# Value products of the rest tiles by chunk with both column halves side by side, and one-row products last in a transform piece

## The chip, the cores and the metric

The kernel runs on one core of one Trainium2 chip. The metric is the device time of one execution in microseconds, lower is better. The kernel before takes 1379.33 us, the median of three runs (1378.09 to 1381.95).

## What is computed

The reference chains three layers on float32 data, for a batch of 4, 8 heads, 576 tokens, a head dimension of 64 and a model dimension of 512:

```python
scores = q @ k.T / 8                      # top 32 scores of each row are kept, the rest masked
attn   = exp(scores - max) masked, divided by its row sum
x      = attn @ v                         # (4, 576, 512) after the heads are joined
mixed  = real(fft over width (fft over tokens (x)))
u      = x + mixed
un     = layer_norm(u);  x2 = u + relu(un @ w_ch1) @ w_ch2
xn     = layer_norm(x2) * g_ln;  out = x2 + relu(xn @ w2_ch1) @ w2_ch2
```

## The kernel before, in words

The order of all work is written out by hand in **slots** `s`. Each of the 144 slots below `TILES` handles one score tile; 36 of them (`NT`) make one batch element `b`. Per slot TensorE transposes the masked exponentials of its tile (`probs_T`, L667), computes later scores (L625, L619), and, where a tile closes a pair, multiplies probabilities by values (`values`). After slot 39 the two-layer MLP is woven in: a unit is one 128-wide slice of the hidden layer, with `mlp1` (L719) and `mlp2` (L736). From slot 144 on only MLP units and the last batch element's transform are left.

VectorE finds the 32nd largest score of each row (`pair`: four rounds of MAX8, L1109, and three of MATCH_REPLACE8, L1115, for two tiles at a time, then the masking multiply L1122), and the next pair starts when the last is done. ScalarE copies PSUM out, computes the exponentials (L902), and issues the loads of scores that were set aside (`sc_ahead`). `probs_T(s)` waits for the mask of its tile; `exps` of a later pair stands behind `probs_out(s)` in ScalarE's order. So VectorE waits for TensorE through ScalarE, and TensorE waits for VectorE at L667.

576 tokens are four full chunks of 128 and a **rest** of 64. Most tiles hold 128 query rows. A **rest tile** (`tile_of(i)` gives chunk `CF`) holds the 64 rest rows of two heads, one head in each half of the partitions. There is one for each pair of heads and batch element, 16 in all, in slots 8, 9, 26, 27 of each batch element's 36: slots 8, 9, 26, 27, 44, 45, 62, 63, 80, 81, 98, 99, 116, 117, 134 and 135. Its value products (L684) take the probabilities as weights, 64 columns for one head, and the values as the moving operand, 65 columns (64 and a column of ones, which yields the row sum). The output `PV` has head 0 in partitions 0 to 63 and head 1 in 64 to 127: each product fills one **column half** of the array. The loop is over heads outside and the five chunks inside, and the fifth chunk is cut to its 64 rows, `pT[0:w]` and `vn[0:w]`. Below those rows `ex` holds zeros (a memset of columns 576 to 639), so `pT` does too, and `vn` holds ones there.

All other tiles use L690, which goes by chunk outside and head inside; its weights are `vn` with 64 columns, its moving operand `pT` with 128 columns, and its output also has one head in each column half.

The transform over tokens and width comes in `PIECES` = 10 pieces per batch element (`dft_piece`): 0 to 3 over tokens (L763, L770), 4 to 9 over width (L775, L779), two for each of three blocks of rows `j`. For batch elements 1 and 2 a piece has two sides of 129 columns, for 0 and 3 one side of 258. Even width pieces (4, 6, 8) add the alternating term, a product with a single contraction row (L779), between the two full products of each side. Pieces come two to a slot: for b = 1 the pieces 4, 6, 8 are in slots 80, 81, 82, for b = 2 in 118, 119, 120, for b = 3 in 152, 153, 154. The even piece stands ahead of `values(s)`, the odd one behind `mlp2`. For b = 0 all pieces come in one burst in slot 37. The third block has 64 rows, so its weights have 64 columns.

In the trace each of these float32 products is two records of a weight load and two of a matmul (transposes are one each), so L684 has 10 products and 20 matmul records for each rest tile.

Of the kernel before, what the change touches and what calls it, by code (L numbers as in the profile page):

```python
# [8 lines left out]
P = 128  # L9
CF = S // P  # L10
TAIL = S - CF * P
C = CF + 1
# [123 lines left out]
def width(c):  # L136

    return P if c < CF else TAIL


def tile_of(i):

    block, r = divmod(i, 2 * TPP)
    if r < 2 * CF:
        return 2 * block, r // 2, r % 2
    if r < 2 * CF + 2:
        return 2 * block + r - 2 * CF, CF, None
    return 2 * block + 1, (r - 2 * CF - 2) // 2, r % 2


def first_tile(hp):

    return hp // 2 * 2 * TPP + (TPP if hp % 2 else 0)


def chunk(b, c):

    return b // 2 * 2 * CF + b // 2 + (2 * CF if c == CF else b % 2 * CF + c)


def piece_slot(b, i):

    if b == 0:
        return SEAM
    return {1: 78, 2: 116, 3: 148}[b] + i // 2
# [42 lines left out]
def build(nc, q, k, v, g2, w_raw, seq_t, wid_t, alt_t, w_low, sc_ahead, out):  # L208
# [4 lines left out]
    with ctx:  # L213
        def sb(name, shape, dt=f32):
            return ctx.enter_context(nc.sbuf_tensor(name, shape, dt))
# [13 lines left out]
        alt = sb("alt", [1, EO])  # L229
        gb = sb("gb", [P, DM])  # L230
        vn = sb("vn", [P, 2, C, 2, D + 1])
# [8 lines left out]
        pT = sb("pT", [P, 2, C * P])  # L240
# [7 lines left out]
        aT = sb("aT", [P, 4, SO])  # L248
# [23 lines left out]
        PV = Tp[:, C * P:C * P + D + 1]  # L272
# [94 lines left out]
        def rest(b):  # L367

            return slice(TAIL * (b % 2), TAIL * (b % 2 + 1))
# [5 lines left out]
        def piece_cols(b, i):  # L375

            total = SO if i < 4 else EO
            return 2 if 0 < b < B - 1 else 1, total // 2 if 0 < b < B - 1 else total

        def piece(b, i):  # L380

            rows = piece_rows(b, i)
            sides, n = piece_cols(b, i)
            if b == 0:
                bank = Ac[rows, i % 4, :] if i % 4 < 3 else Hp[rows, :]
                return bank[:, 0:n].unsqueeze(1)
            if b < B - 1:
                return Sp[rows, :, HALF:HALF + n]
            return Sp[rows, 1, 0:n].unsqueeze(1)
# [215 lines left out]
        def _(pe):  # L605
# [64 lines left out]
            def values(s):  # L670
                b, i = divmod(s, NT)
                hp, t, head = tile_of(i)
                par = hp % 2
                if head == 0:
                    return
                if i <= first_tile(hp) + 1:
                    pe.wait_ge(s_v[par], 3 * 16 * ((NHP // 2) * b + hp // 2 + 1))
                pe.wait_ge(s_pT_sb, s + 1)
                if t == CF:
                    for h in range(2):  # L680
                        o = slice(h * TAIL, (h + 1) * TAIL)
                        for c in range(C):
                            w = width(c)
                            last = nc.tensor.matmul(PV[o, :], pT[0:w, i % 2, c * P + o.start:c * P + o.stop],  # L684
                                                    vn[0:w, par, c, h, :], start=(c == 0), stop=(c == C - 1))
                    last.then_inc(s_pv_ps, 1)
                    return
                for c in range(C):
                    for h in range(2):
                        last = nc.tensor.matmul(OT[h * D:(h + 1) * D, :], vn[:, par, c, h, 0:D], pT[:, h, c * P:(c + 1) * P],  # L690
                                                start=(c == 0), stop=(c == C - 1))
                last.then_inc(s_pv_ps, 2)
# [50 lines left out]
            def dft_piece(b, i):  # L743
                if i == 0:
                    pe.wait_ge(s_fold, b + 1)
                    if b in (1, 2):
                        pe.wait_ge(s_rem, b)
                if b == 0:
                    if i == 0:
                        pe.wait_ge(s_ah_sb, AHEAD)  # L750
                    if i >= 4:
                        pe.wait_ge(s_pc_sb, max(4, i - 3))
                else:
                    pe.wait_ge(s_pc_sb, PIECES * b + i)
                    if b < B - 1:
                        pe.wait_ge(s_sc_sb, min(piece_slot(b, i) + RING + 1, KEPT))
                where, (sides, n) = piece(b, i), piece_cols(b, i)
                for side in range(sides):
                    o, col = where[:, side, :], slice(side * n, (side + 1) * n)
                    if i < 4:  # L760
                        for kc in range(J):
                            r = slice(0, P) if kc < HP else rest(b)
                            last = nc.tensor.matmul(o, xf[r, kc, i // 2, (i % 2) * P:(i % 2 + 1) * P], seq[r, i // 2, kc, col],  # L763
                                                    start=(kc == 0), stop=(kc == J - 1))
                            if i == 2 and kc == 0:

                                for km in range(J):
                                    r = slice(0, P) if km < HP else rest(b)
                                    mid = xs[:, 0, km, FOLD:FOLD + 1] if km < HP else U[r, chunk(b, CF), FOLD:FOLD + 1]
                                    nc.tensor.matmul(o[0:1, :], mid, seq[r, 0, km, col], start=False, stop=False)  # L770
                    else:
                        j, part = divmod(i - 4, 2)
                        to = slice(j * P, j * P + (P if j < HP else TAIL))
                        for kk in range(2):
                            last = nc.tensor.matmul(o, aT[:, 2 * part + kk, to], wid[:, part, kk, col],  # L775
                                                    start=(kk == 0), stop=(kk == 1))
                            if part == 0 and kk == 0:

                                nc.tensor.matmul(o, aT[0:1, 2, to], alt[0:1, col], start=False, stop=False)  # L779
                last.then_inc(s_pc_ps, 1)  # L780

            def un_T(t):
# [26 lines left out]
            for s in range(SLOTS):  # L809
# [19 lines left out]
                if s != SEAM and pieces:  # L829
                    dft_piece(*pieces[0])  # L830
                if s < TILES:
                    values(s)
                for n in closing_at(s):
                    mlp2(n)
                if s != SEAM and pieces:
                    dft_piece(*pieces[1])
# [7 lines left out]
                if s == SEAM:  # L844
                    pe.wait_ge(s_tab, 48)
                    for b, i in pieces:
                        dft_piece(b, i)
# [511 lines left out]
```

## Time and profile before

| | |
|---|---|
| median of three runs | 1379.33 us (1378.09 to 1381.95) |
| profiled execution, its own time | 1380.66 us |
| its span | 1378.9 us |
| TensorE matmul busy | 1271.3 us (92%), 7944 records |
| VectorE busy | 1113.0 us (81%) |
| ScalarE busy | 789.3 us (57%) |
| GpSimd busy | 348.8 us (25%) |
| chain that ended last | TensorE 62%, VectorE 30% |
| mean granted clock of TensorE | 0.971 of full |

How to read it: busy shares are averages over stages that differ, so a saving on TensorE counts only in a stage in which TensorE is what the others wait for. In the rows, `128*64 128x65` means 128 contraction rows by 64 weight columns, and a moving operand of 65 columns. A row of the timeline joins records of one line that follow each other; its time runs from the first start to the last end.

### The profile page before, as it was taken

Reading aid. Unit: us, or ns where it says so; the run is one execution under the profiler, and the core shown is the slowest. Engines: PE = TensorE matmul, PEld = TensorE weight load, DVE = VectorE, ACT = ScalarE, POOL = GpSimd, SP = SyncE. Lnnn points to the kernel's source line nnn. Section 1 sums busy time; section 2 is a strip of 40 time slices with the busy share of each in tenths; the row PEclk is TensorE's granted clock in tenths of the full one; section 3 lists DMA queues with packets and bytes.
Section 4 is the critical chain, followed back from the end, with each engine's and each line's share of the span. In section 5 each row is a group of like instructions: output and inputs, shape, how many; then the busy total and the mean of one; then the engine's idle time right before and its main releaser. Section 6 shows DMA issues by size and latency. Waiting matters only on the chain.

```text
span 1378.9 us, 22760 instructions
## 1 busy us (share of the span) xinstructions
PE 1271.3 (92%) x7944; PEld 1037.2 (75%) x7944; DVE 1113.0 (81%) x2224; ACT 789.3 (57%) x1564; POOL 348.8 (25%) x308
## 2 busy tenths in 40 slices
PE   5877778999999699799998999999999999999999
PEld 2444444777777578688887788888689999999998
DVE  7999999999999988999889789975485555555553
ACT  4777765677777456575665556654344434444442
POOL 3444430122122341132233222322121121212110
PEclk8998989999999999999999999999999999999999
DMA  7899993566757656787786467663244343333342
GB/s 258 310 339 340 328 340 129 186 218 207 245 180 257 191 187 216 247 272 237 231 281 225 155 230 243 218 229 131 76 165 143 121 156 120 130 123 123 122 146 84
DMA packets 117396, 280.63 MB, mean 204 GB/s; under 512 B 29730, under 2 KB 29731, under 8 KB 117283
## 3 DMA queue, kind: packets, MB, share of 16 engines
q1 hardware_dynamic: 105522, 231.98, 51.0%
q10 hardware_dynamic: 10368, 42.47, 8.1%
q0 software_dynamic: 1392, 4.73, 1.0%
q8 instruction: 65, 1.06, 0.3%
q14 instruction: 49, 0.39, 0.1%
HBM read 235.87 MB, written 42.73 MB: 202 GB/s over the span
## 4 chain that ended last, share of the span: by engine, by line
PE 62%; DVE 30%; issue 4%; POOL 1%; ACT 1%; DMA 1%; SPq 0%; DVEq 0%; ACTq 0%; POOLq 0%
PE Big L736 24%; PE Big L719 17%; DVE top L1109 13%; DVE wk L1115 12%; PE Sp L719 7%; PE Tp L667 3%; DVE ex L1122 3%; PE Tp L690 2%; PE Sp L763 2%; PE Tp L684 1%; PE Sp L775 1%; DVE st L1201 1%; PE Tp L794 1%; PE Sp L625 1%; PE Big L763 1%
## 5 line engine op out<-in xcount | busy, mean ns | idle before, releaser
L736 PE MATMUL Big<-wr,hh 128*128 128x512 f32 x1152 | 362.6, 396 | 0.0
L719 PE MATMUL Big<-uh,wr 128*128 128x256 f32 (+1 forms) x1384 | 317.2, 319 | 7.4 <-ACT hh L963 7.4
L1109 DVE MAX8 top<-wk 128x8 f32<-128x576 f32 x432 | 304.4, 746 | 0.0
L719 PEld LDWEIGHTS Big<-uh,wr 128*128 128x128 f32 x1384 | 233.0, 191 | 26.8 <-issue 18.7
L736 PEld LDWEIGHTS Big<-wr,hh 128*128 128x128 f32 x1152 | 217.9, 189 | 41.7
L736 PE MATMUL Big<-wr,hl 128*128 128x512 f32 x576 | 238.3, 414 | 3.6 <-DVE wr L1254 2.6
L500 POOL TENSOR_TENSOR hl<-hf,hh 128x256 fp32r<-128x256 f32 (+1 forms) x123 | 105.3, 856 | 471.7 <-ACT hh L963 471.6
L719 PE MATMUL Big<-ul,wr 128*128 128x256 f32 (+1 forms) x692 | 215.5, 311 | 0.0
L1115 DVE MATCH_REPLACE8 wk<-top,wk 128x576 f32<-128x576 f32 x288 | 211.5, 741 | 0.0
L667 PE MATMUL Tp<-ident,ex 128*128 128x128 f32 x720 | 120.8, 295 | 50.5 <-DVE ex L1122 46.7
L909 ACT ACTIVATE pT<-Tp 128x640 f32<-128x640 f32 x144 | 101.4, 704 | 112.3 <-PE Tp L667 112.0
L667 PEld LDWEIGHTS Tp<-ident,ex 128*128 128x128 f32 x720 | 89.7, 150 | 94.1 <-issue 60.7
L963 ACT ACTIVATE hh<-Big 128x256 fp32r<-128x256 f32 (+1 forms) x173 | 74.6, 431 | 119.1 <-PE Big L719 119.1
L1122 DVE SCALAR_TENSOR_TENSOR ex<-sc,top,ex 128x576 f32<-128x576 f32 x144 | 119.7, 869 | 25.6 <-ACT ex L902 25.6
L719 PEld LDWEIGHTS Big<-ul,wr 128*128 128x128 f32 x692 | 132.5, 192 | 0.0
L736 PEld LDWEIGHTS Big<-wr,hl 128*128 128x128 f32 x576 | 108.8, 189 | 31.1 <-issue 10.8
L1109 DVE MAX8 top<-sc 128x8 f32<-128x576 f32 x144 | 101.6, 747 | 20.5 <-DMA sc<-sc_ahead 13.5
L1115 DVE MATCH_REPLACE8 wk<-top,sc 128x576 f32<-128x576 f32 x144 | 105.7, 741 | 0.0
L902 ACT ACTIVATE ex<-sc,nmx 128x576 f32<-128x576 f32 x144 | 103.9, 769 | 2.3
L494 POOL TENSOR_TENSOR wr<-wf,wr 128x1024 fp32r<-128x1024 f32 x32 | 75.3, 2369 | 111.3 <-DVE top L1109 110.6
L719 PE MATMUL Sp<-uh,wr 128*128 128x384 f32 (+1 forms) x408 | 99.9, 329 | 0.0
L962 ACT ACTIVATE hf<-Big 128x256 f32<-128x256 f32 (+1 forms) x123 | 50.8, 413 | 74.2 <-PE Big L719 74.2
(133 smaller groups left out, 1859.3 us busy)
## 6 DMA issues: line engine op xcount, KB each, us to landing
wf<-in_weights SPq DMA_DIRECT2D x206, 512.0 KB, 3.6
wr<-w_low SPq DMA_DIRECT2D x246, 256.0 KB, 4.3
sc<-in_weights SPq DMA_DIRECT2D x50, 512.0 KB, 3.3
sc<-sc_ahead ACTq DMA_DIRECT2D x36, 576.0 KB, 5.5
w_low<-wr SPq DMA_DIRECT2D x32, 512.0 KB, 6.5
sc_ahead<-U ACTq DMA_DIRECT2D x18, 576.0 KB, 4.7
sc_ahead<-un ACTq DMA_DIRECT2D x9, 576.0 KB, 4.0
sc_ahead<-yb ACTq DMA_DIRECT2D x9, 576.0 KB, 6.3
```

What stands on the lines that cost most here:

```text
L494: pool.tensor_tensor(wr[:, r, :, 1, :], wf[:, j % WFS, :, :], wr[:, r, :, 0, :].bitcast(f32), ALU.subtract).then_inc(s_wlow, 1)
L500: pool.tensor_tensor(hl[:, n % 2, 0:w], hf[:, n % 2, 0:w], hh[:, n % 2, 0:w].bitcast(f32), ALU.subtract).then_inc(s_hl[0], 1)
L667: last = nc.tensor.transpose(Tp[:, c * P:(c + 1) * P], ex[:, s % RING, c * P:(c + 1) * P], ident[:, :])
L719: last = nc.tensor.matmul(hidden(n), a[:, kd * P:(kd + 1) * P], x[:, kd, 0:P * SIZE[p]], start=(kd == 0 and j == 0), stop=(kd == KD - 1 an ...
L736: last = nc.tensor.matmul(Ac[:, j, :], a[:, n % 2, j * P:(j + 1) * P], w, start=(f == 0 and m == 0), stop=(f == KF - 1 and m == 2))
L902: nc.scalar.activation(ex[:, s % RING, 0:S], sc[:, s % RING, :], ACT.Exp, bias=nmx[:, s % RING:s % RING + 1], scale=1.0 / np.sqrt(D)).then ...
L909: nc.scalar.activation(pT[:, s % 2, :], Tp[:, 0:C * P], ACT.Copy).then_inc(s_pT_sb, 1)
L962: nc.scalar.activation(hf[:, n % 2, 0:w], hidden(n), ACT.Relu)
L963: nc.scalar.activation(hh[:, n % 2, 0:w], hidden(n), ACT.Relu).then_inc(s_h_sb, 1)
L1109: nc.vector.max(top[:, s % RING, r, :], src).then_inc(s_top, 1)
L1115: nc.vector.match_replace(out=wk[:, a, :], in_to_replace=top[:, s % RING, r, :], in_values=src, imm_value=STRUCK).then_inc(s_struck, 1)
L1122: nc.vector.scalar_tensor_tensor(out=ex[:, s % RING, 0:S], in0=sc[:, s % RING, :], scalar=top[:, s % RING, ROUNDS - 1, 7:8], in1=ex[:, s % ...
```

## The change

The rest tiles' value products now go by chunk outside and head inside, and all five chunks use 128 rows. The one-row products of an even width piece come after all full products of both sides; the full products of part 0 no longer close their sum, the one-row product does.

```diff
                 if t == CF:
-                    for h in range(2):
-                        o = slice(h * TAIL, (h + 1) * TAIL)
-                        for c in range(C):
-                            w = width(c)
-                            last = nc.tensor.matmul(PV[o, :], pT[0:w, i % 2, c * P + o.start:c * P + o.stop],
-                                                    vn[0:w, par, c, h, :], start=(c == 0), stop=(c == C - 1))
+                    for c in range(C):
+                        for h in range(2):
+                            o = slice(h * TAIL, (h + 1) * TAIL)
+                            last = nc.tensor.matmul(PV[o, :], pT[:, i % 2, c * P + o.start:c * P + o.stop],
+                                                    vn[:, par, c, h, :], start=(c == 0), stop=(c == C - 1))
                     last.then_inc(s_pv_ps, 1)
                     return
...
                         for kk in range(2):
                             last = nc.tensor.matmul(o, aT[:, 2 * part + kk, to], wid[:, part, kk, col],
-                                                    start=(kk == 0), stop=(kk == 1))
-                            if part == 0 and kk == 0:
-
-                                nc.tensor.matmul(o, aT[0:1, 2, to], alt[0:1, col], start=False, stop=False)
+                                                    start=(kk == 0), stop=(kk == 1 and part == 1))
+                if i >= 4 and (i - 4) % 2 == 0:
+                    for side in range(sides):
+                        col = slice(side * n, (side + 1) * n)
+                        last = nc.tensor.matmul(where[:, side, :], aT[0:1, 2, to], alt[0:1, col], start=False, stop=True)
                 last.then_inc(s_pc_ps, 1)
```

Only TensorE's order changes; the instructions of the other four engines are the same and in the same order. The new lines shift the numbers: L684 becomes L683, L690 L689, L719 L718, L736 L735, L775 L774.

First place: TensorE in slot 80, piece 4 of b = 1 with the rest tile behind it, before:

```order
L719 MATMUL Big<-ul,wr 128x256
L775 MATMUL Sp<-wid,aT 128x129
L779 MATMUL Sp<-alt,aT 128x129
L775 MATMUL Sp<-wid,aT 128x129 x2
L779 MATMUL Sp<-alt,aT 128x129
L775 MATMUL Sp<-wid,aT 128x129
L684 MATMUL Tp<-vn,pT 64x65 x10
L736 MATMUL Big<-wr,hl 128x512
```

The same place with the change:

```order
L718 MATMUL Big<-ul,wr 128x256
L774 MATMUL Sp<-wid,aT 128x129 x4
L779 MATMUL Sp<-alt,aT 128x129 x2
L683 MATMUL Tp<-vn,pT 64x65 x10
L735 MATMUL Big<-wr,hl 128x512
```

The two one-row products have moved from between the full products to behind them; the ten products of the rest tile are as many as before, in another order among themselves, which these rows don't tell apart.

Second place: TensorE in slot 118, piece 4 of b = 2, where no value products follow, before:

```order
L794 MATMUL Tp<-ident,un 128x128 x4
L775 MATMUL Sp<-wid,aT 128x129
L779 MATMUL Sp<-alt,aT 128x129
L775 MATMUL Sp<-wid,aT 128x129 x2
L779 MATMUL Sp<-alt,aT 128x129
L775 MATMUL Sp<-wid,aT 128x129
L736 MATMUL Big<-wr,hl 128x512
```

With the change:

```order
L793 MATMUL Tp<-ident,un 128x128 x4
L774 MATMUL Sp<-wid,aT 128x129 x4
L779 MATMUL Sp<-alt,aT 128x129 x2
L735 MATMUL Big<-wr,hl 128x512
```

Here the one-row products now stand directly ahead of `mlp2`, where a full product stood before.

## Rows read from the trace of the kernel before

**Rows 1.** Busy time per stretch: length, PE, PEld, DVE, ACT, POOL, granted clock, DMA share, GB/s.

```profile
0.00:246.00 246.00, 182.52 (x1191) 109.07 (x1191) 235.25 (x504) 163.95 (x262) 80.02 (x46) 0.90 0.82 289
300.00:500.00 200.00, 182.42 (x1317) 145.74 (x1316) 199.15 (x425) 137.88 (x298) 60.21 (x64) 0.97 0.67 217
500.00:560.00 60.00, 60.00 (x428) 48.70 (x429) 48.61 (x102) 33.55 (x75) 11.36 (x14) 1.00 0.63 212
560.00:620.00 60.00, 51.04 (x359) 44.27 (x358) 58.76 (x127) 39.11 (x85) 15.62 (x16) 0.94 0.75 249
620.00:700.00 80.00, 79.62 (x525) 69.28 (x524) 69.72 (x148) 50.47 (x107) 24.36 (x24) 1.00 0.75 244
700.00:825.00 125.00, 116.46 (x793) 97.39 (x792) 110.97 (x237) 72.38 (x158) 38.83 (x38) 0.96 0.64 216
825.00:940.00 115.00, 115.00 (x744) 99.96 (x743) 97.48 (x206) 72.21 (x148) 34.41 (x34) 1.00 0.71 232
940.00:1379.00 439.00, 431.56 (x2219) 380.55 (x2217) 241.86 (x375) 181.86 (x353) 73.85 (x59) 1.00 0.37 123
```

**Rows 2.** Line L684: its busy share in 40 slices of 34.5 us, in tenths.

```profile
busy tenths in 40 slices 0220400040040004004002200400000000000000
```

**Rows 3.** Waits of DVE, three stretches (500:560, 640:700, 750:825): total us, times, longest.

```profile
DVE ex L1122 <- ACT ex L902: 10.6, 2, 6.0
...
DVE top L1109 <- DMA sc<-sc_ahead: 8.1, 3, 4.1
...
DVE ex L1122 <- ACT ex L902: 12.2, 3, 6.0
```

**Rows 4.** Waits of PE, two stretches (560:620, 705:750).

```profile
PE Tp L667 <- DVE ex L1122: 7.4, 2, 5.4
...
PE Tp L667 <- DVE ex L1122: 4.7, 2, 3.5
```

**Rows 5.** Groups by line and shape, L684: count, busy us, mean ns, idle before.

```profile
L684 PE MATMUL Tp<-vn,pT 128*64 128x65 f32 x256 | 21.7, 228 | 0.6 <-ACT pT L909 0.4
L684 PE MATMUL Tp<-vn,pT 64*64 64x65 f32 x64 | 10.4, 243 | 0.0
```

**Rows 6.** Timeline of PE, slot 62: the rest tile's first seven, eight, nine records.

```profile
398.39 0.62 PE L684 MATMUL Tp<-vn,pT 128*64 128x65 f32 x7
...
398.39 0.68 PE L684 MATMUL Tp<-vn,pT 128*64 128x65 f32 x8
...
398.39 0.88 PE L684 MATMUL Tp<-vn,pT 128*64 128x65 f32 x9
```

**Rows 7.** Timeline, slot 83: L690's first two loads; first two, four, all matmul records.

```profile
541.26 0.14 PEld L690 LDWEIGHTS Tp<-pT,vn 128*64 128x64 f32 x2
...
541.26 0.33 PE L690 MATMUL Tp<-pT,vn 128*64 128x128 f32 x2
...
541.26 0.44 PE L690 MATMUL Tp<-pT,vn 128*64 128x128 f32 x4
...
541.26 1.31 PE L690 MATMUL Tp<-pT,vn 128*64 128x128 f32 x20
```

**Rows 8.** Timeline of PE, slots 80 and 82: pieces 4 and 5, a rest tile, piece 8.

```profile
518.12 0.48 PE L779 MATMUL Sp<-alt,aT 1*128 1x129 f32 x2
518.53 0.71 PE L775 MATMUL Sp<-wid,aT 128*128 128x129 f32 x4
519.17 0.48 PE L779 MATMUL Sp<-alt,aT 1*128 1x129 f32 x2
...
520.01 1.80 PE L684 MATMUL Tp<-vn,pT 128*64 128x65 f32 x20
523.25 1.05 PE L775 MATMUL Sp<-wid,aT 128*128 128x129 f32 x8
...
534.84 0.43 PE L779 MATMUL Sp<-alt,aT 1*64 1x129 f32 x2
...
535.79 0.43 PE L779 MATMUL Sp<-alt,aT 1*64 1x129 f32 x2
```

## The prediction

> **What bounds the kernel now.** I read the stretches first, then who waits for whom in each, then the inside of the touched groups. The stretches [rows 1] show two regimes. To 500 us VectorE sets the pace: busy 235.25 of 246 us and 199.15 of 200, while TensorE has room (182.52 and 182.42). The same holds in 560 to 620 (VectorE 58.76 of 60). In 500 to 560, 620 to 700 and 825 to 940 TensorE is busy 60.00 of 60, 79.62 of 80 and 115.00 of 115, and VectorE falls idle. 700 to 825 holds both: first VectorE leads, then TensorE. From 940 on TensorE is busy 431.56 of 439. The waits say the same from the other side. Where TensorE leads, VectorE waits at the mask for ScalarE's exponentials, or for set-aside scores whose load ScalarE issues late: 10.6, 8.1 and 12.2 us [rows 3]. Both stand in ScalarE's order behind a copy of this slot's transposes, so TensorE's lateness is what is passed on. Where VectorE leads, TensorE waits at L667 for the mask, 7.4 and 4.7 us [rows 4].
>
> The 16 rest tiles lie in slices 1, 2, 4, 8, 11, 15, 18, 21, 22 and 25 [rows 2]. Those to slice 11 are the eight of slots 8 to 63, before 414 us, under VectorE's pace. The other eight stand ahead of or in a stretch led by TensorE: slots 80 and 81 (517 to 530 us), 98 and 99, 116 and 117, 134 and 135.
>
> **The rest tile, step by step.** One tile now takes 1.80 us from its first matmul record to the last end [rows 8]. Records of one column half follow each other at 0.06 us (0.62 for seven, 0.68 for eight). The ninth, the first with 64 rows, ends at 0.88 [rows 6]; with a length of 0.27 it starts at 0.61, where the eighth started at 0.68 - 0.22 = 0.46. So a change of the array's row shape costs 0.15 instead of 0.06. The load of the next record also comes out from under its neighbour, another 0.05: 0.14 in all. There are three inside a tile (into 64 rows, out, in again) and one at its end, which stays as a change of another kind. One head's ten records without a shape change would start their last at 0.46 + 2 x 0.06 = 0.58 and end at 0.80.
>
> Do both heads run in that same time? The trace has no 65-column products that alternate between halves; the nearest is L690 with 128 columns, also 64 weight columns a half, also into one PSUM bank [rows 7]. Its first two loads span 0.14 us together, which is one load's length, its first two matmuls 0.33, where two in a row would need 0.11 more, and two more are done 0.11 later. The halves load and stream at once. The step of 0.11 is what 128 columns need in each half: full-width products with 129 columns step by 0.11 too (eight in 1.05, the last about 0.27 long) [rows 8]. 65 columns need half, the 0.06 seen. I therefore take 0.80 us for the tile, a saving of **1.00 us**. The 64 more rows of the fifth chunk cost nothing: the 128-row records are no longer than the 64-row ones (228 against 243 ns) [rows 5]. Bounds: 0.43 (only the three shape changes go, 3 x 0.14) and 1.00. I take the upper, since the half-by-half overlap is seen, and only its rate at 65 columns is not.
>
> The Trainium skill has a rule against this: "TensorE: Matmul & The Clock Gate", Part 3 on packing small matmuls, says that a weight load overlaps matmuls in flight only if its row group differs. Both column halves use all rows, so by that rule the sum would keep at most the shape changes. The trace disagrees: L690's two halves load together on the same rows, and the measurement decides.
>
> **The one-row products.** In piece 4 of slot 80 the first records of the two one-row products are 519.17 - 518.12 = 1.05 us apart, for six records [rows 8]. At the 0.11 of an undisturbed piece (523.25, eight records) these are 0.66, so two shape changes cost 0.39, or **0.195** each. With 64 weight columns (piece 8) it is 535.79 - 534.84 = 0.95, so 0.145 each. A two-sided piece has four such changes inside and now has one inside and one at its exit. The exit before was free only where a 128-column `mlp2` follows a 128-column piece. Saved changes: slots 80, 81, 119: three each at 0.195; slot 118: two; slots 82 and 120 (piece 8): three each at 0.145; b = 3: none in 152 and 153 (two before, two after), one in 154, 0.15; b = 0: none.
>
> **What reaches the end.** A gain passes if a wait on TensorE follows before VectorE takes over.
> - Slots 8 to 63: eight tiles, 8.0 us of TensorE work, nothing. Cover: VectorE, 99.6% busy in 300 to 500. Were it gone, they would add up to 8 us.
> - Slots 80 and 81: 2 x 1.00 + 2 x 0.585 = 3.2 us. Of VectorE's two waits there, 6.0 and 4.6 us, the later stands behind slot 82's transposes: 4.6 is longer than the gain; after it VectorE leads to 620, now 3.2 us earlier. The 0.44 of slot 82 stands behind that wait and is lost.
> - Slots 98 and 99: 2.0 us. VectorE waits 8.1 us for scores afterwards, so it has room.
> - Slots 116 to 120: 2.0 + 0.39 + 0.585 + 0.44 = 3.4 us, under waits of 12.2.
> - Slots 134, 135 and 154: 2.15 us, nothing waits for VectorE for long there.
>
> Sum: 8 x 1.00 for tiles and 2 x 0.585 + 0.39 + 0.585 + 0.44 + 0.15 = 2.7 for one-row products, **10.7 us**. Against the profiled execution's 1380.66 (its span is 1378.9) that gives 1370.0. The median is 1.3 lower, so I forecast 1379.3 - 10.7 = **1368.6 us**. What is late next is VectorE's pair after 84 and 126, and then the same chain. No other engine's order changes, and no wait is added: the piece's semaphore comes earlier, as does that of the tile.
>
> **Rivals.**
> - *The halves do not reach the step of 0.06.* TensorE has then to issue four records in 0.06 us, where L690 never needs more than four in 0.11. If issue caps it at L690's rate, the tile takes 1.31, saves 0.49, and the sum is 8 x 0.49 + 2.7 = 6.6 us: 1372.7. With the halves one after the other it is 8 x 0.43 + 2.7 = 6.1: 1373.2. Against it: L690 issues load, load, matmul, matmul of both halves within hundredths. The Trainium skill (same page, on the issue floor) states some 62 ns of sequencer time per matmul with hardware decoding off; for 20 records that would be an estimate of 1.24 us and a like outcome, but the trace's 0.06 a record is already at that figure and does not exclude it.
> - *VectorE or GpSimd takes over sooner.* Once TensorE is earlier, a layer norm or a copy sets the pace in one of the four places; the smallest room is slot 80's, 4.6 against 3.2. Losing one whole place costs 2 to 3.4 us: 1370.6 to 1372.
> - *The early tiles count too.* If VectorE's 95.6% before 246 us hides waits on TensorE, up to four tiles add 4 us, or up to 8 with the next four: 1360.6 to 1364.6. Against: in 300 to 500 it has 0.85 us idle in all.
> - *Slower, through the clock.* The granted clock is 0.90, 0.97, 0.94 and 0.96 in the stretches where TensorE idles, and 1.00 where it is full [rows 1]. There are two levels, 1.2 and 2.4 GHz; a mean of 0.96 over 125 us is 10 us at the lower, in which work takes twice as long. Less TensorE work under VectorE's lead may bring more such time, and it costs where TensorE leads, half its length. The gain is gone from 22 us more of it in those stretches on; 30 us would make 1379.3 - 10.7 + 15 = 1383.6. Today those stretches show 1.00.
> - *The change does not do what it says:* the one-sided pieces (b = 0 and 3) are reordered for nothing; that is in the sum.
>
> **How the numbers follow.** About 0.3%, 4.1 us, is what a measurement here can tell from none. Forecast case (8 us or more off, one place slightly short included) 0.68; rate capped 0.17; one place lost 0.08; early tiles 0.05; slower through the clock 0.02. The first four each end below 1375.2 (0.98); 0.06 of it I give to two of them falling together, capped rate and a lost place, which ends near 1375.5. So faster 0.92, same 0.06, slower 0.02. The range takes in the capped case and 1.3 of spread above 1372.7, and cuts the deep end of the early tiles: 1364.5 to 1374.
>
> **What would show it.** L683 per tile: 0.80 us for 20 records (1.31 or 1.37 by the first rival), no 64-row shape left. Slot 80's piece: 12 records followed by the rest tile 0.6 us sooner. VectorE's waits smaller by the sums above: 10.6 to about 7.4, 12.2 to about 9. TensorE's total down by about 19 us, the time by 11. I am wrong if a tile takes over 1.2 us, or if TensorE's waits for the mask grow by more than the eight early tiles' share.

## The result, and the profile after

The changed kernel takes 1366.45 us (median of four, 1365.66 to 1367.29) against 1380.64 for the kernel before in the same session (1378.09 to 1382.14). The ratio is 0.9899, 95% interval 0.9887 to 0.9911: 1.0% faster. The forecast was 10.7 us less, 1368.6 us; 14.2 came. (The forecast started from a median of 1379.33; from there it is 12.9.) The profiled execution took 1367.29 us with a span of 1365.5.

The parts inside the groups did what the steps said. A rest tile and slot 80's piece in the timeline of TensorE after, and the first records of a tile in slot 45 (two, three and six matmul records, two loads):

```profile
515.34 1.05 PE L774 MATMUL Sp<-wid,aT 128*128 128x129 f32 x8
516.32 0.71 PE L779 MATMUL Sp<-alt,aT 1*128 1x129 f32 x4
516.96 0.80 PE L683 MATMUL Tp<-vn,pT 128*64 128x65 f32 x20
...
301.12 0.14 PEld L683 LDWEIGHTS Tp<-vn,pT 128*64 128x64 f32 x2 [0.16 <-issue]
...
301.12 0.28 PE L683 MATMUL Tp<-vn,pT 128*64 128x65 f32 x2
...
301.12 0.33 PE L683 MATMUL Tp<-vn,pT 128*64 128x65 f32 x3
...
301.12 0.40 PE L683 MATMUL Tp<-vn,pT 128*64 128x65 f32 x6
```

20 records now take 0.80 us, where they took 1.80 [rows 8]. Two records of different halves end within 0.28 us, two more pairs are done 0.12 later: a pair each 0.06 us. The slot's piece is eight full records, then four one-row records; from its first start to the rest tile's it takes 1.62 us (515.34 to 516.96), where it took 2.21 (517.80 to 520.01): 0.59 less, three changes at 0.195.

Groups by line and shape after, against [rows 5]: the 64-row form is gone, and the 320 records are busy 12.8 us where they were 32.1 in two rows.

```profile
L683 PE MATMUL Tp<-vn,pT 128*64 128x65 f32 x320 | 12.8, 226 | 0.6 <-ACT pT L909 0.4
```

Busy time per stretch after, in the columns of [rows 1]:

```profile
0.00:246.00 246.00, 175.38 (x1192) 103.47 (x1192) 235.34 (x504) 163.22 (x262) 80.14 (x46) 0.92 0.82 289
300.00:500.00 200.00, 180.68 (x1322) 144.25 (x1320) 199.76 (x426) 138.17 (x298) 60.15 (x64) 0.97 0.66 218
500.00:560.00 60.00, 58.23 (x452) 48.11 (x451) 51.84 (x110) 36.22 (x81) 12.54 (x15) 1.00 0.67 232
700.00:825.00 125.00, 114.05 (x793) 96.75 (x791) 114.33 (x243) 72.43 (x158) 40.87 (x40) 0.99 0.66 220
```

Waits of VectorE after, in the three stretches of [rows 3], and of TensorE in the two of [rows 4]:

```profile
DVE ex L1122 <- ACT ex L902: 7.2, 2, 5.9
...
DVE top L1109 <- DMA sc<-sc_ahead: 8.0, 2, 4.7
...
DVE ex L1122 <- ACT ex L902: 9.0, 3, 5.6
...
PE Tp L667 <- DVE ex L1122: 7.1, 2, 5.4
...
PE Tp L667 <- DVE ex L1122: 5.6, 2, 3.4
```

VectorE's wait at the mask shrank from 10.6 to 7.2 us in 500 to 560, and from 12.2 to 9.0 in 750 to 825: by 3.4 and 3.2, about the gains of slots 80, 81 and 116 to 120. Where the time came from shows in the starts of L667, slot by slot, before less after (the 0.05 by which the traces differ at slot 0 taken off): nothing by slots 36 and 38 (0.0), 2.0 us by slot 46, 2.4 by slot 66 and still 2.4 at slot 80, 5.5 by slot 88, 5.8 by slot 92, 7.7 by slot 100, 11.2 by slot 123, 13.1 by slot 136, 13.3 at the last matmul. The four forecast places gave what they should. The 2.4 us before slot 80 were not forecast.

TensorE's busy total fell by 24.9 us (1271.3 to 1246.4), not by 19. 7.1 us of this lie in the first 246, where four tiles give 4.0 and the granted clock was 0.92 instead of 0.90. Over the span the mean clock was 0.979 instead of 0.971, by estimate from these means some 23 us less at the lower of the two levels.

### The profile page after: what moved, and what is told of

Its sections match the earlier page's. It is cut to its first block, busy times and chain, and to the rows that moved or that the text cites. A ratio compares the mean times of both kernels' runs of the same rounds, so it can differ in the third digit from the quotient of the medians.

```text
span 1365.5 us, 22760 instructions
## 1 busy us (share of the span) xinstructions
PE 1246.4 (91%) x7944; PEld 1018.9 (75%) x7944; DVE 1111.1 (81%) x2224; ACT 787.8 (58%) x1564; POOL 350.0 (26%) x308
## 4 chain that ended last, share of the span: by engine, by line
PE 62%; DVE 31%; issue 4%; POOL 1%; ACT 1%; DMA 1%; SPq 0%; DVEq 0%; ACTq 0%; POOLq 0%
PE Big L735 24%; PE Big L718 17%; DVE top L1109 13%; DVE wk L1115 12%; PE Sp L718 7%; PE Tp L667 3%; DVE ex L1122 3%; PE Tp L689 2%; PE Sp L762 2%; PE Sp L774 1%; PE Tp L794 1%; DVE st L1201 1%; PE Sp L625 1%; PE Big L762 1%; PE Tp L683 1%
## 5 line engine op out<-in xcount | busy, mean ns | idle before, releaser
L735 PE MATMUL Big<-wr,hh 128*128 128x512 f32 x1152 | 362.1, 395 | 0.0
L718 PE MATMUL Big<-uh,wr 128*128 128x256 f32 (+1 forms) x1384 | 315.8, 318 | 9.5 <-ACT hh L963 8.9
L718 PEld LDWEIGHTS Big<-uh,wr 128*128 128x128 f32 x1384 | 231.9, 190 | 29.3 <-issue 20.4
L735 PEld LDWEIGHTS Big<-wr,hh 128*128 128x128 f32 x1152 | 217.4, 189 | 41.5
L735 PE MATMUL Big<-wr,hl 128*128 128x512 f32 x576 | 237.7, 413 | 3.6 <-DVE wr L1254 2.7
L718 PE MATMUL Big<-ul,wr 128*128 128x256 f32 (+1 forms) x692 | 214.9, 311 | 0.0
L667 PE MATMUL Tp<-ident,ex 128*128 128x128 f32 x720 | 117.6, 290 | 54.3 <-DVE ex L1122 49.0
L667 PEld LDWEIGHTS Tp<-ident,ex 128*128 128x128 f32 x720 | 87.1, 147 | 96.4 <-issue 62.1
L735 PEld LDWEIGHTS Big<-wr,hl 128*128 128x128 f32 x576 | 108.9, 189 | 31.8 <-issue 11.3
L718 PEld LDWEIGHTS Big<-ul,wr 128*128 128x128 f32 x692 | 131.8, 190 | 0.0
L718 PE MATMUL Sp<-uh,wr 128*128 128x384 f32 (+1 forms) x408 | 100.0, 329 | 0.0
L689 PE MATMUL Tp<-pT,vn 128*64 128x128 f32 x1280 | 86.4, 283 | 11.8 <-ACT pT L909 11.5
```

What stands on the lines that cost most here:

```text
L667: last = nc.tensor.transpose(Tp[:, c * P:(c + 1) * P], ex[:, s % RING, c * P:(c + 1) * P], ident[:, :])
L718: last = nc.tensor.matmul(hidden(n), a[:, kd * P:(kd + 1) * P], x[:, kd, 0:P * SIZE[p]], start=(kd == 0 and j == 0), stop=(kd == KD - 1 an ...
L735: last = nc.tensor.matmul(Ac[:, j, :], a[:, n % 2, j * P:(j + 1) * P], w, start=(f == 0 and m == 0), stop=(f == KF - 1 and m == 2))
```

## Experiments

All are built from the kernel before or after with the edit shown. Gains are against the kernel before of the same session.

**The tiles alone.** The kernel before with the change's first piece of diff only.

> Only the rest tiles' value products in the new form, the one-row products as before. My theory: a tile takes 0.80 us instead of 1.80; the eight late tiles give 8.0 us, and the four of slots 44 to 63 give the 2.4 us by which the changed kernel was ahead at slot 80: 10.4 us less than before. Rival (VectorE hides all early tiles): 8.0 us less.

1369.47 us against 1380.35, ratio 0.9913 (0.9898 to 0.9929), 10.9 us less. The interval, 9.8 to 14.1 us, holds the 10.4 and leaves out the rival's 8.0.

**The one-row products alone.** The second piece only.

> Only the one-row products moved to the end of a piece, the tiles as before. Both theories: 2.7 us less than before (0.2 us for each array-shape change saved in slots 80, 81, 118 to 120 and 154), nothing changed before slot 80. If the parts need each other, this plus the tiles alone falls short of the whole by more than 1 us.

1376.95, ratio 0.9977 (0.9966 to 0.9988), 3.4 us less. The two parts sum to 14.3, the whole gave 14.2: as far as medians with intervals of 1.5 to 2 us either way can tell, they do not need each other.

**Early and late tiles apart.**

```diff
                 if t == CF:
-                    for h in range(2):
-                        o = slice(h * TAIL, (h + 1) * TAIL)
+                    if s < 72:
                         for c in range(C):
...
+                            for h in range(2):
...
+                    else:
+                        for h in range(2):
...
```

That is the early one, with the change's loop in the first branch and the old one in the second; the late one has `s >= 72`.

> The new form only in the eight rest tiles of slots 8 to 63, everything else as before. My theory: 2.4 us less than before, none of it by slot 38, 2.0 by slot 58, 2.4 by slot 66, and then it stays to the end, since VectorE was not full there though it showed 99.6% busy. Rival (VectorE sets the pace, the gain is swallowed): within 0.5 us of before.

> The new form only in the eight rest tiles of slots 80 to 135. My theory and the forecast's sum: 8.0 us less than before (2.0 at each of the four places). Rival (a place is swallowed by VectorE when it comes alone): 6.0 or less.

Early: 1377.36, ratio 0.9979 (0.9967 to 0.9991), 3.0 us less. Late: 1371.13, ratio 0.9929 (0.9914 to 0.9944), 9.2 less against 8.0. Each of the four late places gave 2.0 us in the starts of L667. The early tiles' interval is 1.2 to 4.6 us, so they do reach the end, against the forecast, though VectorE shows 99% busy there. Only slots 44, 45, 62 and 63 count: at slot 36 their trace is level with that of before. (At slot 38 it is 0.5 us behind, and that of the late tiles, whose work up to there is that of before, 0.6 ahead: traces scatter by that much.)

**What shape changes cost.**

The heads side by side with the fifth chunk still cut:

```diff
-                    for h in range(2):
-                        o = slice(h * TAIL, (h + 1) * TAIL)
-                        for c in range(C):
-                            w = width(c)
+                    for c in range(C):
+                        w = width(c)
+                        for h in range(2):
+                            o = slice(h * TAIL, (h + 1) * TAIL)
```

And full rows with the heads one after the other:

```diff
-                            w = width(c)
-                            last = nc.tensor.matmul(PV[o, :], pT[0:w, i % 2, c * P + o.start:c * P + o.stop],
-                                                    vn[0:w, par, c, h, :], start=(c == 0), stop=(c == C - 1))
+                            last = nc.tensor.matmul(PV[o, :], pT[:, i % 2, c * P + o.start:c * P + o.stop],
+                                                    vn[:, par, c, h, :], start=(c == 0), stop=(c == C - 1))
```

> The heads side by side, but the fifth chunk still cut to its 64 rows (one-row products as before). My theory: one array-shape change stays inside the tile, so it takes 0.80 + 0.14 = 0.94 us and the kernel is 8 x 0.14 = 1.1 us slower than with the tiles' whole change alone. Rival (side by side needs full rows to overlap): 1.3 us or more for a tile.

> Full rows in the fifth chunk, but one head after the other as before (one-row products as before). My theory: only the three shape changes go, a tile takes 1.80 - 0.42 = 1.38 us, the kernel is 3.4 us faster than before by the late tiles, and up to 1 more by the early ones. Rival (full rows cost streaming time): over 1.5 us for a tile.

The rest tile of slot 62 in the timeline of the first, and in that of the second:

```profile
396.68 0.95 PE L684 MATMUL Tp<-vn,pT 128*64 128x65 f32 x20
```

```profile
397.35 1.20 PE L683 MATMUL Tp<-vn,pT 128*64 128x65 f32 x20
```

Cut rows side by side: 0.95 us, one shape change of 0.15 inside, as expected; 1371.64 us, ratio 0.9933 (0.9918 to 0.9948). Full rows one after the other: 1.20, not 1.38; 1373.4, ratio 0.9947 (0.9932 to 0.9962). My 1.38 took the second head's records to start after the first's. With no shape change between them the second half's first records run beside the first half's last: its first matmul starts 0.17 us before the first half's last one does. So full rows alone give 0.60 of a tile's 1.00 us and the order by chunk the other 0.40; taken the other way, the order alone gives 0.85 and full rows 0.15. In the starts of L667 a late place of two tiles gave 1.7 us with cut rows (slots 80, 98 and 134; at 116 only 0.15, where 3.4 us of its trace are at the lower clock and none before) and 1.2 with full rows (all four). Both totals lie off what was expected: the first is 2.2 us behind the tiles alone, a run of another session, for 1.1 expected; the second is 7.3 us faster than before, for 3.4 to 4.4, as its tile took 1.20.

**Is VectorE full in 246 to 500 us?** In the kernel before, the mask of slot 49 lasts 1.82 us instead of 0.80. VectorE (masks) and GpSimd in its timeline:

```profile
310.63 0.80 DVE L1122 SCALAR_TENSOR_TENSOR ex<-sc,top,ex 128x576 f32<-128x576 f32 x1
310.69 1.87 POOL L507 TENSOR_TENSOR ul<-uf,uh 128x512 fp32r<-128x512 f32 x1 [0.23 <-ACT uf L953]
...
311.36 1.82 DVE L1122 SCALAR_TENSOR_TENSOR ex<-sc,top,ex 128x576 f32<-128x576 f32 x1
```

GpSimd's subtraction starts inside the first mask and lasts 1.87 us. The second mask starts in the middle of it and ends at 313.18, 0.62 us after the subtraction's end, a little less than a mask's own length. I cut the subtraction to 8 of its 128 columns (the MLP's low part is left out for the rest), with old and with new early tiles.

```diff
+            pool.memset(ul[:, 1, :, :].bitcast(f32), 0.0)
+            pool.memset(ul[:, 0, :, 2 * P:].bitcast(f32), 0.0)
...
-                pool.tensor_tensor(ul[:, p % 2, :, cs], uf[:, t % 2, :, :], uh[:, p % 2, :, cs].bitcast(f32),
+                cs = slice(j * P, j * P + 8)
+                pool.tensor_tensor(ul[:, p % 2, :, cs], uf[:, t % 2, :, 0:8], uh[:, p % 2, :, cs].bitcast(f32),
```

> The kernel before, with GpSimd's subtraction that makes the low part of the transposed activations cut to 8 of 128 columns (for all groups after the first; the rest of that buffer stays zero or old, so the MLP's low part is left out there). It tests the collision: masks of VectorE that last 1.0 to 1.8 us instead of 0.8, each beside that subtraction. My theory: no mask over 0.9 us between 246 and 500 us, VectorE's chain 1.6 us earlier by slot 66 with TensorE's tiles unchanged. Rival (the long masks are waits for TensorE or ScalarE written as busy time): they stay as long.

> As the one before (the same subtraction cut), with the new form in the eight rest tiles of slots 8 to 63. My theory: since no collision is left to be avoided, the early tiles give only the 0.7 us of VectorE's true waits for a copy of scores, against the kernel with the same cut and old tiles. Rival (the early gain is a wait on TensorE in full): 2.4 us.

The two masks of slots 48 and 49 with the small subtraction and old tiles:

```profile
310.03 0.80 DVE L1125 SCALAR_TENSOR_TENSOR ex<-sc,top,ex 128x576 f32<-128x576 f32 x1
310.10 0.85 POOL L510 TENSOR_TENSOR ul<-uf,uh 128x32 fp32r<-128x32 f32 x1 [0.23 <-ACT uf L956]
...
310.76 0.81 DVE L1125 SCALAR_TENSOR_TENSOR ex<-sc,top,ex 128x576 f32<-128x576 f32 x1
```

The long mask is gone: it was the collision with GpSimd. Others stayed (1.3 us in slots 54 and 58), so "no mask over 0.9" was a miss. The question is what it is worth. Starts of slots 44 and 60 (the transposes, L667 or its shifted line) in the timelines of before, of small subtraction with old tiles, and of small subtraction with new early tiles:

```profile
292.45 0.92 PE L667 MATMUL Tp<-ident,ex 128*128 128x128 f32 x5
...
383.29 0.74 PE L667 MATMUL Tp<-ident,ex 128*128 128x128 f32 x5 [0.59 <-DVE ex L1122]
```

```profile
291.86 0.92 PE L670 MATMUL Tp<-ident,ex 128*128 128x128 f32 x5
...
382.69 0.74 PE L670 MATMUL Tp<-ident,ex 128*128 128x128 f32 x5 [0.59 <-DVE ex L1125]
```

```profile
291.83 0.92 PE L670 MATMUL Tp<-ident,ex 128*128 128x128 f32 x5
...
380.68 0.74 PE L670 MATMUL Tp<-ident,ex 128*128 128x128 f32 x5 [0.59 <-DVE ex L1132]
```

The stretch takes 90.84 us before, 90.83 without the collision, 88.85 with new tiles too. Taking away VectorE's lost microsecond gave nothing; the tiles gave all their 2.0. Both halves of my theory on the collision fall here (1.6 for its removal, 0.7 left for the tiles), the rival holds: before the change TensorE leads in slots 44 to 57. In VectorE's waits of 290 to 420 us most of the lost time comes back as waiting, before, and with the small subtraction (another 0.3 is the mask of slot 54, 1.05 us before and 1.32 here):

```profile
DVE top L1109 <- ACT sc L868: 0.7, 2, 0.5
```

```profile
DVE top L1112 <- ACT sc L871: 1.3, 3, 0.7
```

The totals were 1378.31 with old tiles (ratio 0.9984, 0.9974 to 0.9993) and 1373.25 with new ones (0.9949, 0.9934 to 0.9964). Their 5 us also hold slots 62 and 63 and the granted clock (below), so I read the stretch and not the total.

**More work instead of less.** The value products of two rest tiles done twice, in the kernel before.

```diff
-                    for h in range(2):
+                    for _ in range(2 if s in (44, 45) else 1):
+                        for h in range(2):
...
```

The other kernel has (62, 63).

> The kernel before with the value products of the rest tiles of slots 44 and 45 done twice (the second time they overwrite the first), 1.8 us more TensorE work in each. My theory (TensorE leads in slots 44 to 57, and VectorE's 99% is partly masks stretched beside GpSimd): 3.6 us later by slot 58 and at the end. Rival (VectorE leads there, as the forecast had it): within 0.5 us by slot 62.

> The same doubling in the rest tiles of slots 62 and 63. My theory: here VectorE leads (TensorE waits for the mask in slots 60, 62, 66, 70, 72 and 74), so the 3.6 us are swallowed: within 0.5 us of before by slot 74. Rival (TensorE leads here too): 3.6 us later.

Starts of slots 44 and 60 with the doubling in 44 and 45, then VectorE's waits in 290 to 420 us:

```profile
292.42 0.92 PE L667 MATMUL Tp<-ident,ex 128*128 128x128 f32 x5
...
386.78 0.73 PE L667 MATMUL Tp<-ident,ex 128*128 128x128 f32 x5 [0.59 <-DVE ex L1123]
...
DVE top L1110 <- ACT sc L869: 4.9, 3, 2.4
```

94.36 us instead of 90.84: all of the 3.5 us pass, and VectorE's wait grows from 0.7 to 4.9. The total is 1383.45, ratio 1.0022 (1.0012 to 1.0031), 2.8 more. With 62 and 63 doubled, the starts of slots 62 and 74, before and in this run, then two masks and VectorE's waits in 400 to 475 us of this run:

```profile
395.42 0.74 PE L667 MATMUL Tp<-ident,ex 128*128 128x128 f32 x5 [0.43 <-DVE ex L1122]
...
467.41 0.74 PE L667 MATMUL Tp<-ident,ex 128*128 128x128 f32 x5 [2.14 <-DVE ex L1122]
...
395.96 0.74 PE L667 MATMUL Tp<-ident,ex 128*128 128x128 f32 x5 [0.43 <-DVE ex L1123]
...
469.91 0.74 PE L667 MATMUL Tp<-ident,ex 128*128 128x128 f32 x5 [2.15 <-DVE ex L1123]
...
429.50 1.28 DVE L1123 SCALAR_TENSOR_TENSOR ex<-sc,top,ex 128x576 f32<-128x576 f32 x1
...
442.06 1.28 DVE L1123 SCALAR_TENSOR_TENSOR ex<-sc,top,ex 128x576 f32<-128x576 f32 x1
...
DVE top L1110 <- ACT sc L869: 1.2, 2, 0.9
```

73.95 us, against 467.41 - 395.42 = 71.99 before: 1.96 of 3.6 pass, where I expected under 0.5. Two masks (slots 69 and 71) that were 0.81 long before are now 1.28, each beside a GpSimd operation; that is 0.9 us of it. VectorE also waits 1.2 us for ScalarE's copies of scores, where it waited for nothing in that stretch before, and the mask of slot 64 is 0.4 shorter: 1.8 in sum. The total does not resolve it: 1381.19, ratio 1.0004 (0.9994 to 1.0013).

**How much of a saving passes.** VectorE's slack in the kernel before accounts for it: its waits, and the time by which its masks are stretched. Between the masks of slots 44 and 60 it waited 0.65 us, and the masks of slots 49 and 54 were 1.27 us longer together than the others: 1.9 us. In the traces of the change and of the early tiles neither is left, and 2.0 us came. With the small subtraction it is 1.3 of waits and 0.5 of stretch (slot 54) before the new tiles, nothing with them, and 2.0 again. Behind slots 62 and 63 there is only the mask of slot 64, 1.16 us before and 0.79 after, and 0.4 came. This is arithmetic on the traces: no run takes a saving larger than the slack. Nor is every stretched mask slack: those of slots 58, 60 and 62 (1.31, 1.13 and 1.82 us) are about as long after the change. After the change VectorE has no slack left in slots 44 to 57, and that a further saving on TensorE there would pass is not shown. TensorE still reaches L667 there 2 to 11 us after the mask, so being late at that wait does not by itself show who leads.

**A version that goes further.** If shape changes are dear, the token pieces have them too: 128-row, one-column and 64-row products mixed, side after side.

```diff
-                    if i < 4:
-                        for kc in range(J):
...
+                if i < 4:
+                    for kcs, kms in ((range(HP), range(HP)), (range(HP, J), range(HP, J))):
+                        def chunks():
+                            for side in range(sides):
...
+                        def middles():
+                            for side in range(sides if i == 2 else 0):
...
+                        if kcs[0] == 0:
+                            last = chunks()
+                            middles()
+                        else:
+                            middles()
+                            last = chunks()
```

> The changed kernel with the token pieces (0 to 3) ordered in the same manner: the 128-row products of both sides, then the one-column middle products, then the 64-row products. It saves two array-shape changes in a two-sided piece and six in piece 2, so 12 for each of the batch elements 1 and 2 and one for 3. My theory (a shape change is dear and TensorE leads in slots 78, 79, 116 and 117): at 0.15 to 0.2 us each, 3.7 to 4.9 us less than the changed kernel, so about 18 less than before. Rival (VectorE takes over once TensorE is that early): 2 us or less.

1360.7 us (1360.56 to 1361.69), ratio 0.986 (0.9845 to 0.9874): 19.9 us less than before, the fastest kernel of this study. The first piece of slot 78 in the trace after, and in this one:

```profile
495.09 2.38 PE L762 MATMUL Sp<-seq,xf 128*128 128x160 f32 x12
```

```profile
493.69 1.99 PE L767 MATMUL Sp<-seq,xf 128*128 128x160 f32 x12
```

The 12 records take 0.39 us less, with two shape changes fewer. From slot 78 to 80 it gains 2.1 us on the changed kernel and from 116 to 118 2.15, 12 changes each: 0.18 a change. That is 4.3 us of its 5.7. In the two traces another 1.6 us comes between slots 74 and 78, where the granted clock differs (below).

## Why the prediction was right, and where it was off

- **The rest tile, 1.80 to 0.80 us:** right to the hundredth, in all 16 tiles. The halves load and stream side by side at the step of 0.06. The rival of a capped rate is refuted by the same rows. So is, for these column halves, the Trainium skill's rule on row groups ("TensorE: Matmul & The Clock Gate", Part 3): two loads on the same rows span 0.14 us together while the first matmul is in flight.
- **The shape change:** 0.14 inside a tile (measured 0.15 with cut rows), 0.195 in a piece (0.18 and 0.195 in the further version). Right. Missed: between two halves of one shape there is also an overlap of 0.17, seen with full rows alone. It did not enter the sum, but it makes the lower bound of a tile's saving 0.60, not 0.43 (and 3 x 0.14 is 0.42).
- **The four late places:** 3.2, 2.0, 3.4 and 2.15 us forecast; the starts of L667 show 3.1, 2.0, 3.4 and 2.0 (slot 154's 0.15 comes behind the last of them), with 0.3 to 0.4 in small steps beside them. Slot 82's 0.4 came and was lost again by slot 88, as forecast. Right.
- **"Slots 8 to 63: nothing. Cover: VectorE, 99.6% busy in 300 to 500":** this step failed, for four of the eight tiles. 2.0 us of slots 44 and 45 and 0.4 of 62 and 63 arrived. The "early tiles count too" rival had it, with a chance of 0.05 and the price of 4 to 8 us too high; its own counter-argument, 0.85 us idle, was the wrong reading. I took busy time for the lead. VectorE had 0.7 us of waits in 290 to 420, and two masks (slots 49 and 54) stretched by 1.3 us in all, which filled time in which it would have waited: together the 2.0 us that passed. The sign in the trace was that up to slot 57 TensorE comes to L667 3 to 12 us after the mask is ready, so it never waits for VectorE there, and only from slot 60 does it; how much would pass, VectorE's slack said. Slots 8 to 27, where TensorE did wait in every pair, gave 0.0, as forecast.
- **The sum:** 10.7 + 2.4 = 13.1, against 13.3 in the traces and 14.2 in the medians. The forecast range held it, though the cover over the early tiles was wrong. The remainder is within the interval of the measured ratio, 12.3 to 15.6 us. That the median landed in the range with 2.4 us missed is in part because the range is wide, 9.5 us.
- **The clock rival:** nothing was given back; the mean granted clock rose from 0.971 to 0.979.

## What to carry to other kernels

Among short float32 products, look at what stands between them: each change of the array's rows or columns cost 0.14 to 0.2 us here, two to three ordinary steps (0.06 and 0.11), so products of one shape belong together, and padding with zero rows cost less than a change. Where each output takes half of the array's columns, alternate the halves: here both ran in 0.80 us, the time worked out for one. An engine at 99% busy need not lead: look at its waits and at instructions of it that are longer than their like. What of these was gone after the change was the size of what came back from the other engine (2.0 and 0.4 us here). Adding work to the other engine shows whether it has slack itself, not how much a saving would return.

## What was unexpected in the hardware

**Busy time that is waiting.** VectorE's mask reads two operands from SBUF, and beside a GpSimd operation it lasted 1.82 us in slot 49 instead of 0.80, booked as busy. With the GpSimd operation cut short, it was 0.81. The Trainium skill says this in "SBUF — State Buffer", under who interferes with whom: a VectorE instruction with two SBUF inputs and a GpSimd instruction that reads SBUF block each other fully, whoever comes second waiting to the other's end. The rows agree: the subtraction, started inside the first mask, lasts 1.87 us where the one of the same slot after lasts 1.28, and the second mask ends 0.6 us after the subtraction.

**Two us from the granted clock.** From slot 76 to 78 the traces of before and after take 13.0 and 13.1 us, that of the early tiles 10.9 (480.54 to 491.48). Three others (late tiles, full rows, 62 and 63 doubled) take 13.0 to 13.1, the remaining seven 9.8 to 10.9. The granted clock in the stretch 484 to 492 us, before and with the early tiles:

```profile
484.00:492.00 8.00, 5.73 (x30) 4.84 (x30) 8.00 (x16) 4.93 (x11) 6.75 (x6) 0.79 0.68 221
```

```profile
484.00:492.00 8.00, 7.33 (x58) 6.15 (x58) 8.00 (x18) 5.26 (x13) 6.77 (x8) 1.00 0.69 239
```

A mean of 0.79 over 8 us is 3.4 us at the lower level, 1.2 GHz; in the other it stayed at 2.4 GHz. Before it TensorE had idled in both, 6.5 and 5.8 of the 17 us from 470 to 487, and why only one falls again is not shown. The work there is the same. This alone moves a profiled execution by 2 us, the size of a small term of the sum, which is why the terms were read slot by slot.
